# An attention and two gated layers on one core: the take of step 3 by halves, an earlier release of head B's tail, and the waits for values in another place

## The chip, the core and the metric

One core of one Trainium2 chip. Its engines work side by side: TensorE (matrix products into PSUM), VectorE, ScalarE, GpSimd, and SyncE, which issues the DMAs. They are kept in order by semaphores that the program sets and waits for. The metric is the device time in microseconds of one execution; lower is better. PSUM has 8 banks of 512 float32 for each of the 128 partitions.

## The reference

Three layers. The first takes almost half of the time and is the one that the change touches.

```python
q_pool = q.reshape(B, H, S // 2, 2, D).mean(axis=3)     # B 4, H 8, S 1152, D 64: 576 queries
scores = scale * (q_pool @ k.T)                         # 576 x 1152 a head
attn = exp(scores - max(scores)); attn /= sum(attn) + 1e-9
x = attn @ v
# layer 2: gelu(x @ w_in) split in u and v, v normalized and mixed over tokens, x + (u * v_s) @ w_out
# layer 3: token mixing and channel mixing with relu, both added to x
```

All is float32. Where a product must be exact, each operand is split in a high and a low part, and three products are summed.

## The kernel before, in words

The 32 heads are worked on in 16 pairs, called blocks here (index i, block 0 to 15); the pair's heads are A and B. A head has 576 queries: four tiles of 128 and a tail of 64. The two tails of a pair make one tile together, so a block has 9 tiles, one for each step s: steps 0 to 3 are the tiles of head A, step 4 (TAIL_STEP) is the joint tail, steps 5 to 8 are the tiles of head B. Blocks 1 to 14 run in a hardware loop whose body holds two of them on TensorE; block 15 is written out, and so is a rest of four steps, called block 16 here.

In each step TensorE does three things in this order (`step` in the TensorE program, L780):

- 18 transposes (L704, `transpose_p`) of the normalized probabilities of the tile that is 4 steps back (LAG), into banks 4 to 6. They wait until GpSimd has normalized that tile and until ScalarE and VectorE have copied the previous transposes out of the banks.
- The product with V (L775, `values`) for the pair before, spread over the steps by PV_STEPS: blocks of 128 keys, 9 for head A in steps 0 to 3 (3, 2, 2, 2) and 9 for head B in steps 4 to 8 (1, 2, 2, 2, 2). Each block of keys is two matmuls, each of which shows as two passes. They sum up in bank 7.
- The scores of this step's tile (`scores`, L759, and for the tail L742 to L744) into banks 0 to 3, 288 keys a bank. They wait for `s_taken`: VectorE has taken the scores of the step before out of these banks. For the tail there are 12 matmuls over the whole array, three for each bank in turn, elsewhere 24 on half of it, two at a time.

VectorE has in each step: the copy of half of the transposes (L1329, `evac_p`), the reciprocal of the sum of the tile two steps back (L1320, L1322), and the take (L1313, `take`): one operation of 128x1152 that scales the scores, writes them to `prob` and reduces them to the negated row maximum in `nmax`; the accumulated value is written by a small second instruction, which also reports `s_taken`. ScalarE copies the other half of the transposes and those of the last block of keys (L1081), does the exponential with `nmax` as bias (L1095) and copies the sums of the value product to `xT`. GpSimd normalizes (L592) and prepares q and k of the next block (L552 to L585); late in blocks 13 to 15 it also splits the first weights of layer 2. SyncE issues the loads, V among them (L459), and the copies of q and k to the other half of the partitions.

The transposed probabilities `pT` are held once for each head. Before they are overwritten, `pT_free` (L425) waits for `acc_ready`, which the last block of keys in `values` reports. For the tail of head B, in step 8, both VectorE (all blocks of keys but the last) and ScalarE (the last) wait in this way.

The first block of keys in a head's `values` stands behind four waits: the accumulator is copied out (`acc_moved`), the transposes of all tiles of the head are copied by VectorE and by ScalarE (`pT_by_dve`, `pT_by_act`), and V is there (`v_in`). In the loop the counts of such waits depend on the block and are worked out by instructions of TensorE's queue.

In block 0, steps 0 to 3 use the banks 0 to 3 and 4 to 7 in turn, and the transposes of its step 4 wait for all four takes.

Of the kernel before, what the change touches and what calls it, by code (L numbers as in the profile page):

```python
# [54 lines left out]
def build(nc, q, k, v, x_w_in, g_ln, w_sg, b_sg, w_out, w_tok1, w_tok2, w_ch1, w_ch2, out):  # L55
# [49 lines left out]
    def sem(name):  # L105
        return top.enter_context(nc.semaphore(name))

    with top:
# [31 lines left out]
        ctx0.close()  # L140
        pT = sb(ctx1, "pT", [P, 2, KB, SQ])
        nmax = sb(ctx1, "nmax", [P, NS])
        esum = sb(ctx1, "esum", [P, NS])
        lsum = sb(ctx1, "lsum", [P, NS])
        rsum = sb(ctx1, "rsum", [P, NS])
# [88 lines left out]

        s_ready = sem("s_ready")
        s_taken = sem("s_taken")
        exp_done = sem("exp_done")
        lsum_ready = sem("lsum_ready")
        rsum_ready = sem("rsum_ready")
# [2 lines left out]
        pT_by_act = sem("pT_by_act")  # L242
        pT_by_dve = sem("pT_by_dve")
        acc_ready = sem("acc_ready")
        acc_moved = sem("acc_moved")

        sgT_hi = sem("sgT_hi")
# [435 lines left out]
        def _(pe):  # L683
# [39 lines left out]
            def scores(i, par, s, first):  # L723

                zero = isinstance(i, int) and i == 0
                if s == (TAIL_STEP if zero else 0):
                    pe.wait_ge(q_split, at(i, 1, 1))
                    pe.wait_ge(k_split, at(i, 1, 1))
                if s == 0 and not zero:
                    pe.wait_ge(over_put[0], at(i, 64, 0))  # L730
                if s == TAIL_STEP + 1:
                    pe.wait_ge(over_put[1], at(i, 64, 64))
                if first and s < LAG:
                    if s >= 2:
                        pe.wait_ge(s_taken, s - 1)
                else:
                    pe.wait_ge(s_taken, at(i, NS, s))
                if s == TAIL_STEP:
                    tail = slice(4 * P, QC)
                    for c in range(SCORE_BANKS):  # L740
                        cols = slice(c * CK, (c + 1) * CK)
                        te.matmul(ps[:, c, 0:CK], qh2[:, par, tail], kh2[:, par, cols], start=True, stop=False)  # L742
                        te.matmul(ps[:, c, 0:CK], qh2[:, par, tail], kl2[:, par, cols], start=False, stop=False)  # L743
                        ins = te.matmul(ps[:, c, 0:CK], ql2[:, par, tail], kh2[:, par, cols], start=False, stop=True)  # L744
                        if c >= 2:
                            ins.then_inc(s_ready, 1)
                    return
                a, q0 = head_of(s), tile_of(s) * P
                b0 = first_bank(s) if first else 0
                for m in range(2):  # L750
                    if s == 0 and zero:
                        pe.wait_ge(two_split, 2 + m)
                    if s == 2 and zero:
                        pe.wait_ge(q_rest_split, 1)
                    for term in range(3):
                        for t in range(2):
                            wh, wl, xh, xl = row_tile(i, a, t, par, q0, 2 * m + t)
                            w, x = ((wh, xh), (wh, xl), (wl, xh))[term]
                            ins = te.matmul(ps[:, b0 + 2 * m + t, 0:CK], w, x, start=(term == 0), stop=(term == 2))  # L759
                            if m == 1 and term == 2:  # L760
                                ins.then_inc(s_ready, 1)

            def values(i, a, js):

                if js[0] == 0:
                    if not (isinstance(i, int) and i + a == 0):
                        pe.wait_ge(acc_moved, at(i, 4, 2 * a))
                    last = TAIL_STEP if a == 0 else NS - 1
                    pe.wait_ge(pT_by_dve, at(i, NS, last + 1))
                    pe.wait_ge(pT_by_act, at(i, 2 * NS, 2 * last + 2))  # L770
                    pe.wait_ge(v_in[a], at(i, 16, 16))
                n = HALF
                for j in js:
                    for c in range(2):
                        ins = te.matmul(ps[PH * c:PH * c + PH, ACC_BANK, 0:n], v_sb[:, a, j, :],  # L775
                                        pT[:, a, j, c * n:c * n + n], start=(j == 0), stop=(j == KB - 1))
                        if j == KB - 1:
                            ins.then_inc(acc_ready, 1)

            def step(i, par, s, first=False, tail=False):  # L780

                if s >= LAG and not tail:
                    if first and s == LAG:
                        pe.wait_ge(s_taken, LAG)
# [168 lines left out]
            pe.wait_ge(w_split, U_WO)  # L953
            v_tile(0, 0)
            v_tile(0, 1)
            for s in range(TAIL_STEP, NS):
                values(NP - 1, *PV_STEPS[s])
            for b in range(B):
# [316 lines left out]
        def _(dve):  # L1275
# [29 lines left out]
            def take(i, s):  # L1305
# [3 lines left out]
                if not (isinstance(i, int) and i + before[0] < 0):  # L1309
                    dve.wait_ge(p_ready, at(i + before[0], 2 * NS, 2 * before[1] + 2))  # L1310
                dve.wait_ge(s_ready, at(i, 2 * NS, 2 * s + 2))
                b0 = first_bank(s) if isinstance(i, int) and i == 0 else 0
                ve.tensor_scalar(prob[:, PROB_BUF[s], :].rearrange("p (c n) -> p c n", c=SCORE_BANKS),  # L1313
                                 ps[:, b0:b0 + SCORE_BANKS, 0:CK], -SCALE, BIG, ALU.mult, ALU.min,
                                 accum_out=nmax[:, s:s + 1]).then_inc(s_taken, 1)
# [8 lines left out]
            def evac_p(i, s):  # L1324

                dve.wait_ge(p_ready, at(i, 2 * NS, 2 * s + 2))
                if s in (0, TAIL_STEP, TAIL_STEP + 1):
                    pT_free(dve, i, head_of(s))
                ve.tensor_copy(pT_of(s, 1), trans(1)).then_inc(pT_by_dve, 1)  # L1329

            def step(i, s, first=False, tail=False):
# [274 lines left out]
```

## Time and profile before

| what | us |
|---|---|
| median of 3 runs | 1007.95 (1007.74 to 1008.92) |
| the profiled execution | 1007.09 |
| its span | 1005.0 |
| TensorE busy in the span | 985.4 (98%), 8898 matmuls |
| VectorE busy | 568.5 (57%) |
| ScalarE busy | 464.0 (46%) |
| GpSimd busy | 382.8 (38%) |

The profiled execution is one, and its span begins and ends a little inside its time. Matmuls overlap one another, so a busy TensorE isn't one without gaps: what counts is when a group of matmuls starts after the one before it. The attention lasts until about 429 us; from there on TensorE works on layers 2 and 3. The granted clock of TensorE is 9 tenths or more in every slice but the first (8 tenths).

### The profile page before, as it was taken

What the parts mean: (1) busy time and instruction counts of PE and PEld (TensorE: products, weight loads), DVE (VectorE), ACT (ScalarE), POOL (GpSimd) and SP (SyncE); (2) the same over time, 40 slices, a digit from 0 to 9 for tenths busy, and PEclk for the clock granted to TensorE, in tenths of its full rate; (3) what the DMA queues carried; (4) which work ended last, traced back from release to release, by engine and by line L of the source; (5) the groups of instructions that cost most, each with busy time, mean ns of one, the idle gap of its engine ahead of it and who ended that gap; (6) DMA issues with size and microseconds to landing.
All of it is one profiled execution on the core that took longest, in us unless ns stands there. A gap on an engine that the chain in (4) does not pass through costs nothing.

```text
span 1005.0 us, 22892 instructions
## 1 busy us (share of the span) xinstructions
PE 985.4 (98%) x8898; PEld 813.9 (81%) x8898; DVE 568.5 (57%) x1125; ACT 464.0 (46%) x880; POOL 382.8 (38%) x297
## 2 busy tenths in 40 slices
PE   6999999999999999999999999999999999999998
PEld 6877777777777777679999999988888888888898
DVE  6777777777777777779484948554213113121121
ACT  4787777777777877754242514222111111111111
POOL 4877777777777777730000104385000000000000
PEclk8999999999999999999999999999999999999999
DMA  5644444444444434310000000142001001000010
GB/s 184 182 119 118 117 117 117 116 112 114 116 117 117 117 91 109 111 55 1 1 2 1 2 1 24 46 135 73 1 0 42 1 1 42 0 15 27 0 42 22
DMA packets 34475, 65.55 MB, mean 65 GB/s; under 512 B 6272, under 2 KB 15360, under 8 KB 34432
## 3 DMA queue, kind: packets, MB, share of 16 engines
q1 hardware_dynamic: 33984, 64.37, 22.5%
q8 instruction: 33, 0.54, 0.2%
q10 hardware_dynamic: 448, 0.56, 0.2%
q14 instruction: 10, 0.08, 0.0%
HBM read 42.93 MB, written 4.72 MB: 47 GB/s over the span
## 4 chain that ended last, share of the span: by engine, by line
PE 92%; issue 2%; DVE 2%; POOL 1%; ACT 1%; DMA 1%; SPq 0%; DVEq 0%; ACTq 0%; POOLq 0%
PE ps L816 18%; PE ps L817 18%; PE ps L818 18%; PE ps L775 14%; PE ps L759 11%; PE ps L704 7%; PE ps L742 1%; DVE prob L1313 1%; PE ps L743 1%; PE ps L744 1%; PE ps L868 1%; DMA k_raw<-in_k 1%; ACT prob L1095 1%; POOL prob L592 0%; PE ps L822 0%
## 5 line engine op out<-in xcount | busy, mean ns | idle before, releaser
L1313 DVE TENSOR_SCALAR_CACHE_REDUCE prob<-ps 128x1152 f32<-128x1152 f32 x144 | 195.4, 1358 | 82.0 <-PE ps L759 62.8
L592 POOL TENSOR_SCALAR prob<-prob,rsum 128x1152 f32<-128x1152 f32 x144 | 178.4, 1239 | 106.0 <-DVE rsum L1322 106.0
L1095 ACT ACTIVATE prob<-prob,nmax 128x1152 f32<-128x1152 f32 x144 | 181.2, 1258 | 5.2
L775 PE MATMUL ps<-pT,v_sb 128*64 128x288 f32 x1152 | 170.6, 418 | 1.3
L1554 DVE SCALAR_TENSOR_TENSOR f_l<-ps,f_h 128x512 fp32r<-128x512 f32 (+1 forms) x60 | 38.3, 638 | 222.4 <-ACT f_h L1262 222.4
L1262 ACT ACTIVATE f_h<-ps 128x512 fp32r<-128x512 f32 (+1 forms) x60 | 33.3, 555 | 254.7 <-PE ps L818 254.7
L1081 ACT ACTIVATE pT<-ps 128x512 f32<-128x512 f32 (+1 forms) x288 | 111.9, 435 | 78.0 <-PE ps L704 69.4
L759 PE MATMUL ps<-k_over,q_over 64*128 64x288 f32 x744 | 131.5, 309 | 0.0
L759 PEld LDWEIGHTS ps<-k_over,q_over 64*128 64x128 f32 x744 | 102.1, 184 | 26.4 <-DVE prob L1313 25.8
L704 PE MATMUL ps<-ident,prob 64*128 64x64 f32 x2592 | 106.8, 224 | 6.7 <-DVE prob L1313 3.9
L704 PEld LDWEIGHTS ps<-ident,prob 64*128 64x128 f32 x2592 | 100.7, 139 | 13.8 <-issue 12.8
L1329 DVE COPY pT<-ps 128x512 f32<-128x512 f32 x144 | 98.9, 687 | 10.3 <-PE ps L775 5.7
L775 PEld LDWEIGHTS ps<-pT,v_sb 128*64 128x64 f32 x1152 | 70.8, 136 | 40.9 <-issue 3.2
L817 PE MATMUL ps<-u_l,c_h 128*128 128x512 f32 (+1 forms) x240 | 88.3, 368 | 0.0
L816 PE MATMUL ps<-u_h,c_h 128*128 128x512 f32 (+1 forms) x240 | 88.3, 368 | 0.0
L818 PE MATMUL ps<-u_h,c_l 128*128 128x512 f32 (+1 forms) x240 | 88.3, 368 | 0.0
L816 PE MATMUL ps<-f_h,c_h 128*128 128x512 f32 (+1 forms) x240 | 88.3, 368 | 0.0
L817 PE MATMUL ps<-f_l,c_h 128*128 128x512 f32 (+1 forms) x240 | 88.3, 368 | 0.0
L818 PE MATMUL ps<-f_h,c_l 128*128 128x512 f32 (+1 forms) x240 | 88.3, 368 | 0.0
L759 PE MATMUL ps<-kh,qh 64*128 64x288 f32 x248 | 85.3, 344 | 0.6 <-DMA k_over<-kl 0.6
L652 POOL TENSOR_TENSOR rstd<-var_e,minus_half 128x1 f32<-128x1 f32 x18 | 13.3, 741 | 167.2 <-DVE var_e L1405 167.2
L759 PE MATMUL ps<-kl,qh 64*128 64x288 f32 x248 | 72.3, 291 | 0.0
(156 smaller groups left out, 2136.9 us busy)
## 6 DMA issues: line engine op xcount, KB each, us to landing
q_raw<-in_q SPq DMA_DIRECT2D x16, 640.0 KB, 5.2
k_raw<-in_k SPq DMA_DIRECT2D x16, 576.0 KB, 4.0
v_sb<-in_v SPq DMA_DIRECT2D x32, 288.0 KB, 2.9
k_over<-kh SPq DMA_DIRECT2D x31, 144.0 KB, 2.5
k_over<-kl SPq DMA_DIRECT2D x31, 144.0 KB, 2.6
out_x<-xT SPq DMA_DIRECT2D x4, 1024.0 KB, 4.2
q_over<-qh SPq DMA_DIRECT2D x31, 128.0 KB, 2.2
q_over<-ql SPq DMA_DIRECT2D x31, 128.0 KB, 2.3
```

The costliest lines, as they stand in the source:

```text
L592: g.tensor_scalar(sl, sl, rsum[:, s:s + 1], 0.0, ALU.mult, ALU.add).then_inc(norm_done, 1)
L704: ins = te.transpose(dst, prob[half, PROB_BUF[s], j * P:(j + 1) * P], ident[half, half])
L759: ins = te.matmul(ps[:, b0 + 2 * m + t, 0:CK], w, x, start=(term == 0), stop=(term == 2))
L775: ins = te.matmul(ps[PH * c:PH * c + PH, ACC_BANK, 0:n], v_sb[:, a, j, :], pT[:, a, j, c * n:c * n + n], start=(j == 0), stop=(j == KB - 1))
L816: te.matmul(acc, wh, xh, start=start, stop=False)
L817: te.matmul(acc, wh, xl, start=False, stop=False)
L818: return te.matmul(acc, wl, xh, start=False, stop=stop)
L1081: return sc.activation(o, i_, ACT.Copy)
L1095: sc.activation(sl, sl, ACT.Exp, scale=-1.0, bias=nmax[:, s:s + 1], accum_out=esum[:, s:s + 1]).then_inc(exp_done, 1)
L1313: ve.tensor_scalar(prob[:, PROB_BUF[s], :].rearrange("p (c n) -> p c n", c=SCORE_BANKS), ps[:, b0:b0 + SCORE_BANKS, 0:CK], -SCALE, BIG, AL ...
L1329: ve.tensor_copy(pT_of(s, 1), trans(1)).then_inc(pT_by_dve, 1)
L1554: ve.scalar_tensor_tensor(out=f_l[:, f % F_N, 0:n], in0=ps[:, f % F_N, 0:n], scalar=0.0, in1=f_h[:, f % F_N, 0:n].bitcast(F32), op0=ALU.ma ...
```

## The change

- The take of step 3 is done in two operations of 128x576, two banks each. Each reports `half_taken` and leaves its own negated maximum in `nmax_half`. VectorE then waits for both and joins them with one scalar operation of 128x1 (the minimum of the two) into `nmax`, which reports `s_taken`.
- The scores of the tail (step 4) no longer wait for `s_taken`; they wait for the first half ahead of bank 0 and for the second ahead of bank 2.
- In step 8 VectorE's copy of the tail of head B waits for `tail_read`, which `values` reports when the eighth block of keys (number 7) of head B is done, and no longer for the ninth. ScalarE's copy waits as before.
- The wait for V of a head stands at the start of step 0 or 4, ahead of the transposes, and the two waits for `pT_by_dve` and `pT_by_act` in `values` are left out; behind the loop, ahead of the last values, the three stand written out.

```diff
--- before.py
+++ after.py
@@ -140,6 +140,7 @@
         ctx0.close()
         pT = sb(ctx1, "pT", [P, 2, KB, SQ])
         nmax = sb(ctx1, "nmax", [P, NS])
+        nmax_half = sb(ctx1, "nmax_half", [P, 2])
         esum = sb(ctx1, "esum", [P, NS])
         lsum = sb(ctx1, "lsum", [P, NS])
         rsum = sb(ctx1, "rsum", [P, NS])
@@ -234,6 +235,7 @@
 
         s_ready = sem("s_ready")
         s_taken = sem("s_taken")
+        half_taken = sem("half_taken")
         exp_done = sem("exp_done")
         lsum_ready = sem("lsum_ready")
         rsum_ready = sem("rsum_ready")
@@ -242,6 +244,7 @@
         pT_by_act = sem("pT_by_act")
         pT_by_dve = sem("pT_by_dve")
         acc_ready = sem("acc_ready")
+        tail_read = sem("tail_read")
         acc_moved = sem("acc_moved")
 
         sgT_hi = sem("sgT_hi")
@@ -733,11 +736,13 @@
                 if first and s < LAG:
                     if s >= 2:
                         pe.wait_ge(s_taken, s - 1)
-                else:
+                elif s != TAIL_STEP:
                     pe.wait_ge(s_taken, at(i, NS, s))
                 if s == TAIL_STEP:
                     tail = slice(4 * P, QC)
                     for c in range(SCORE_BANKS):
+                        if c % 2 == 0:
+                            pe.wait_ge(half_taken, at(i, 2, c // 2 + 1))
                         cols = slice(c * CK, (c + 1) * CK)
                         te.matmul(ps[:, c, 0:CK], qh2[:, par, tail], kh2[:, par, cols], start=True, stop=False)
                         te.matmul(ps[:, c, 0:CK], qh2[:, par, tail], kl2[:, par, cols], start=False, stop=False)
@@ -765,10 +770,6 @@
                 if js[0] == 0:
                     if not (isinstance(i, int) and i + a == 0):
                         pe.wait_ge(acc_moved, at(i, 4, 2 * a))
-                    last = TAIL_STEP if a == 0 else NS - 1
-                    pe.wait_ge(pT_by_dve, at(i, NS, last + 1))
-                    pe.wait_ge(pT_by_act, at(i, 2 * NS, 2 * last + 2))
-                    pe.wait_ge(v_in[a], at(i, 16, 16))
                 n = HALF
                 for j in js:
                     for c in range(2):
@@ -776,9 +777,14 @@
                                         pT[:, a, j, c * n:c * n + n], start=(j == 0), stop=(j == KB - 1))
                         if j == KB - 1:
                             ins.then_inc(acc_ready, 1)
+                        elif j == KB - 2 and a == 1 and c == 1:
+                            ins.then_inc(tail_read, 1)
 
             def step(i, par, s, first=False, tail=False):
 
+
+                if s in (0, TAIL_STEP) and not first:
+                    pe.wait_ge(v_in[s // TAIL_STEP], at(i, 16, 0))
                 if s >= LAG and not tail:
                     if first and s == LAG:
                         pe.wait_ge(s_taken, LAG)
@@ -953,6 +959,9 @@
             pe.wait_ge(w_split, U_WO)
             v_tile(0, 0)
             v_tile(0, 1)
+            pe.wait_ge(pT_by_dve, NP * NS)
+            pe.wait_ge(pT_by_act, NP * 2 * NS)
+            pe.wait_ge(v_in[1], NP * 16)
             for s in range(TAIL_STEP, NS):
                 values(NP - 1, *PV_STEPS[s])
             for b in range(B):
@@ -1310,6 +1319,16 @@
                     dve.wait_ge(p_ready, at(i + before[0], 2 * NS, 2 * before[1] + 2))
                 dve.wait_ge(s_ready, at(i, 2 * NS, 2 * s + 2))
                 b0 = first_bank(s) if isinstance(i, int) and i == 0 else 0
+                if s == TAIL_STEP - 1:
+
+                    for m in range(2):
+                        cols = slice(m * 2 * CK, (m + 1) * 2 * CK)
+                        ve.tensor_scalar(prob[:, PROB_BUF[s], cols].rearrange("p (c n) -> p c n", c=2),
+                                         ps[:, b0 + 2 * m:b0 + 2 * m + 2, 0:CK], -SCALE, BIG, ALU.mult, ALU.min,
+                                         accum_out=nmax_half[:, m:m + 1]).then_inc(half_taken, 1)
+                    dve.wait_ge(half_taken, at(i, 2, 2))
+                    ve.tensor_scalar(nmax[:, s:s + 1], nmax_half[:, 0:1], nmax_half[:, 1:2], None, ALU.min).then_inc(s_taken, 1)
+                    return
                 ve.tensor_scalar(prob[:, PROB_BUF[s], :].rearrange("p (c n) -> p c n", c=SCORE_BANKS),
                                  ps[:, b0:b0 + SCORE_BANKS, 0:CK], -SCALE, BIG, ALU.mult, ALU.min,
                                  accum_out=nmax[:, s:s + 1]).then_inc(s_taken, 1)
@@ -1324,8 +1343,11 @@
             def evac_p(i, s):
 
                 dve.wait_ge(p_ready, at(i, 2 * NS, 2 * s + 2))
-                if s in (0, TAIL_STEP, TAIL_STEP + 1):
+                if s in (0, TAIL_STEP + 1):
                     pT_free(dve, i, head_of(s))
+                if s == TAIL_STEP and not (isinstance(i, int) and i == 0):
+
+                    dve.wait_ge(tail_read, at(i, 1, 0))
                 ve.tensor_copy(pT_of(s, 1), trans(1)).then_inc(pT_by_dve, 1)
 
             def step(i, s, first=False, tail=False):
```

## Rows read from the trace of the kernel before

**Rows 1.** the page, part 4 (the chain that ended last, shares of the span)

```profile
PE 92%; issue 2%; DVE 2%; POOL 1%; ACT 1%; DMA 1%; SPq 0%; DVEq 0%; ACTq 0%; POOLq 0%
```

**Rows 2.** timeline of TensorE, a regular step (start us, us, engine, line, op, tiles)

```profile
207.43 0.40 PE L759 MATMUL ps<-k_over,q_over 64*128 64x288 f32 x1
...
208.33 0.71 PE L704 MATMUL ps<-ident,prob 64*128 64x64 f32 x18
208.98 1.19 PE L775 MATMUL ps<-pT,v_sb 128*64 128x288 f32 x8
210.10 0.40 PE L759 MATMUL ps<-k_over,q_over 64*128 64x288 f32 x1
```

**Rows 3.** timeline of TensorE, steps 3 to 5 of one block

```profile
198.59 0.40 PE L759 MATMUL ps<-kh,qh 64*128 64x288 f32 x1
...
199.49 0.72 PE L704 MATMUL ps<-ident,prob 64*128 64x64 f32 x18
200.34 0.71 PE L775 MATMUL ps<-pT,v_sb 128*64 128x288 f32 x4
201.15 0.40 PE L742 MATMUL ps<-kh,qh 128*128 128x288 f32 x1
...
202.93 0.77 PE L704 MATMUL ps<-ident,prob 64*128 64x64 f32 x18
```

**Rows 4.** timeline of TensorE, step 8 of that block to step 0 of the next

```profile
212.76 0.40 PE L759 MATMUL ps<-k_over,q_over 64*128 64x288 f32 x1
...
213.77 0.77 PE L704 MATMUL ps<-ident,prob 64*128 64x64 f32 x18
214.48 1.68 PE L775 MATMUL ps<-pT,v_sb 128*64 128x288 f32 x12
216.09 0.39 PE L759 MATMUL ps<-kh,qh 64*128 64x288 f32 x1
```

**Rows 5.** timeline of VectorE, steps 3 and 4, and the tail's copy in step 8

```profile
199.73 1.36 DVE L1313 TENSOR_SCALAR_CACHE_REDUCE prob<-ps 128x1152 f32<-128x1152 f32 x1 [0.45 <-PE ps L759]
201.01 0.08 DVE L1313 DVE_READ_ACCUMULATOR prob<-ps 128x1 f32 x1
201.01 0.69 DVE L1329 COPY pT<-ps 128x512 f32<-128x512 f32 x1
201.61 0.15 DVE L1320 TENSOR_SCALAR lsum<-esum 128x1 f32<-128x1 f32 x1
...
203.04 1.36 DVE L1313 TENSOR_SCALAR_CACHE_REDUCE prob<-ps 128x1152 f32<-128x1152 f32 x1 [1.08 <-PE ps L744]
...
212.97 0.69 DVE L1329 COPY pT<-ps 128x512 f32<-128x512 f32 x1 [0.38 <-PE ps L775]
```

**Rows 6.** timeline of TensorE, step 4 of block 15

```profile
407.72 0.40 PE L742 MATMUL ps<-kh,qh 128*128 128x288 f32 x1 [0.29 <-DVE prob L1313]
```

**Rows 7.** list of waits (us in total, times, longest us)

```profile
DVE pT L1329 <- PE ps L775: 5.7, 15, 0.4
```

**Rows 8.** timelines of ScalarE and of GpSimd, in the same block

```profile
201.59 1.26 ACT L1095 ACTIVATE prob<-prob,nmax 128x1152 f32<-128x1152 f32 x1
...
212.91 0.28 ACT L1081 ACTIVATE pT<-ps 128x128 f32<-128x128 f32 x1 [0.53 <-PE ps L775]
...
203.28 1.25 POOL L592 TENSOR_SCALAR prob<-prob,rsum 128x1152 f32<-128x1152 f32 x1
```

**Rows 9.** timeline of SyncE's queue, step 3

```profile
198.87 0.33 SPq L459 DMA_DIRECT2D v_sb<-in_v  x1
```

**Rows 10.** timeline of TensorE, step 0 of block 1

```profile
37.39 0.39 PE L759 MATMUL ps<-kh,qh 64*128 64x288 f32 x1 [0.63 <-DMA k_over<-kl]
```

**Rows 11.** the chain in order of time, block 0 (start us, us, what)

```profile
14.97 1.28 DVE prob L1313 x2
```

**Rows 12.** timelines of GpSimd and of TensorE, block 13 to step 2 of block 14

```profile
367.27 1.23 POOL L592 TENSOR_SCALAR prob<-prob,rsum 128x1152 f32<-128x1152 f32 x1 [0.89 <-DVE rsum L1322]
...
373.82 0.78 PE L704 MATMUL ps<-ident,prob 64*128 64x64 f32 x18 [0.83 <-POOL prob L592]
```

## The prediction

> **What bounds the kernel now.** I read the page first: TensorE holds 92% of the chain that ended last [rows 1], so only TensorE's own gaps are worth anything, and a gap that comes back once per block of the attention counts 15 times (blocks 1 to 15; block 0 is filled differently). The timeline of TensorE shows the regular step: first score matmul 207.43, transposes 208.33, values 208.98, next scores 210.10 [rows 2]. That is 0.90, 0.65 and 1.12, a step of 2.67. Two places in a block leave this grid.
>
> Step 3 to step 4: scores 198.59, transposes 199.49, values 200.34, tail scores 201.15 [rows 3]. Transposes to values is 0.85 instead of 0.65, values to scores 0.81. Step 4 has only 4 value passes: 12 passes take 216.09 - 214.48 = 1.61 [rows 4] where 8 take 1.12 [rows 2], so 4 passes are 0.49 and 4 passes before scores should take 1.12 - 0.49 = 0.63. The whole stretch is 2.56; on the grid it would be 0.90 + 0.65 + 0.63 = 2.18.
>
> Step 8 to step 0: scores 212.76, transposes 213.77, values 214.48 [rows 4]: 1.01 and 0.71 instead of 0.90 and 0.65. The 1.61 behind them is on the grid.
>
> Who holds these gaps? For step 4 VectorE's rows say it: the take of step 3 runs from 199.73, its accumulator read ends at 201.01 + 0.08 = 201.09 [rows 5], and the tail scores start 0.06 later. The four waits in front of the values (0.20 late) are at present covered by it: in block 15 the row of the tail scores names the take as releaser too [rows 6]. Either edit alone would give little or only a part there: without the take the values' waits still cost 0.20. For step 0 it is VectorE's copy of head B's tail at 212.97 [rows 5]: it ends at 213.66, the transposes that overwrite its bank begin at 213.77. The list of waits has that copy held back by a value matmul 15 times, 5.7 us in all [rows 7].
>
> **Take by halves.** 1152 elements occupy VectorE 201.01 - 199.73 = 1.28, 512 occupy it 201.61 - 201.01 = 0.60 [rows 5]: 0.68 for 640, so 1.06 ns each and 0.06 fixed. A half of 576 is then about 0.67 to 0.68. First half: 199.73 + 0.68, its read 0.08, 0.06 to TensorE: 200.55. TensorE wants its banks at 198.59 + 2.18 = 200.77: 0.22 to spare. Second half: 199.73 + 1.36 + 0.08 + 0.06 = 201.23. Bank 2 is wanted after six tail matmuls; twelve and the switch behind them take 202.93 - 201.15 = 1.78 [rows 3], so not before 200.77 + 0.8 = 201.57: 0.34 to spare. If the second half must wait for the first one's read (0.08) both still hold. No row has two accumulating operations back to back; I bound the extra cost of a half from nothing to that of a whole further small operation with its read, 0.06 to 0.3, and take 0.08, which the rows of the copy beside the read show.
>
> The joining operation is a 128x1 one like lsum: 0.15 [rows 5], with its start some 0.18. So the maximum of step 3 is 0.08 + 0.08 + 0.18, at most some 0.35 later, as is all that VectorE does behind it: the copy for step 0's transposes ends at 201.70 + 0.35 = 202.05, and the transposes of step 5 come at 202.93 - 0.38 = 202.55. Behind it the two small operations end by 202.35, the take of step 4 can start no earlier than 203.04 - 0.38 = 202.66 [rows 5]. ScalarE's exponential of step 3 starts at 201.59 before [rows 8], later than the new maximum (201.44). GpSimd's normalization 203.28 to 204.53 [rows 8] sits behind a split that starts from step 3, not from step 4, so it doesn't move; its transposes are two steps on, at 205.66 - 0.38 = 205.28 on the grid. Nothing comes late. Taken with the next edit the stretch goes from 2.56 to 2.18. I take 0.37, a little under the 0.38, for the blocks not shown: 15 x 0.37 = **5.6 off**. The ends for this term: 0.2 (if the halves are 0.17 later than I reckon) to 0.38 a block.
>
> **Waits for values.** The two waits for the transposed blocks are covered, since the transposes of the same step wait for a later copy; the wait for V goes ahead of the transposes, where TensorE's queue is still full of scores. Queued behind it are the transposes. V for head A is issued at 198.87 [rows 9] and lands in 2.9 by the page's median; wanted at 213.6. It never bites. Per wait removed from the short stretch between transposes and values I count the 0.20 above over three, and none left: in block 15, whose counts are constants, nothing of the kind shows before the take's row. Its gain is in the 0.37 already. Alone it is nothing, for the take would still end at 201.09.
>
> **Head B's tail.** VectorE's copy only waits for block 7 of head B. The eight passes of step 8 end at 212.83, and block 8 is the last four of them, 0.49 earlier: 212.35. VectorE is free at 212.59, its read ends there. So the copy starts at about 212.55, 0.42 earlier, and ends at 213.24. Next late would be ScalarE's copy 212.91 to 213.19 [rows 8], which still waits for block 8; the transposes are due at 212.76 + 0.90 = 213.66. So 1.01 becomes 0.90. The 0.06 behind it (transposes that start into an idle array) should go as well: 0.17. At every other boundary the loop branches back and the new wait stands right behind the branch: I take 0.12 there, so 0.15 on average (bounds 0 to 0.22). Not all boundaries pay:
> - Into block 1 it is lost: TensorE then waits 0.63 for a DMA of the k copies [rows 10].
> - Into blocks 2 to 13: 12 x 0.15 = **1.8 off**.
> - Into blocks 14 and 15 TensorE stands later on GpSimd, which splits a weight in between (0.83 before the transposes at 373.82). That chain starts with the normalization at 367.27, for which GpSimd had waited 0.89 on VectorE's reciprocal behind this very copy [rows 12]. A copy 0.42 earlier starts it 0.42 earlier: 2 x 0.42 = **0.8 off**.
> - Into block 16 ScalarE's chain from the end of block 8 decides, which isn't moved: nothing.
>
> **Block 0** has the take of step 3 on its chain (14.97, followed by the preparation of q [rows 11]), and its transposes wait for the whole take in any case: 0.3 longer (0.25 to 0.4), passed on to the scores that wait in [rows 10]: **0.3 on**.
>
> The Trainium skill, "Perfetto Trace Analysis", section "Optimizing Scalar/DVE Operations", gives VectorE some 125 ns of access per instruction that reads PSUM, against the 60 to 80 of the rows. By it each half costs 0.05 more, block 0 loses 0.4 and the sum changes by 0.1; the same section allows breaking up an instruction where the engine has slack but makes another one wait, and here VectorE stands idle for 1.08 before the take at 203.04 [rows 5].
>
> **Sum.** 5.6 + 1.8 + 0.8 - 0.3 = 7.9 off. The profiled execution took 1007.09 (span 1005.0 and 2.1 around it): 999.2. The median of the runs shown is 1007.95, 0.86 above it; with the same distance the time is **1000.1**. Behind the attention everything hangs on its end and shifts as a whole.
>
> **Rivals.**
> 1. The halves come late. For: no row of such a pair, only 0.22 to spare. Against: every part of it has a row. At 0.17 beyond the spare time step 4 gives 0.2: 15 x 0.17 = 2.6 less, **1002.7**. Chance 0.10.
> 2. The tail's edit gives nothing. For: ScalarE's copy of the last block ends at 213.19, and both engines must have reported; the branch. Against: 0.47 lies between it and the transposes on the grid (213.66). Then 1.8 and 0.8 go: **1002.7**. Chance 0.10. If only the boundaries with the branch fail: 1000.9, within my own range.
> 3. It doesn't do what it says: the tail scores start where they did, because their second half's wait or another operand holds them; only the tail's edit counts, less block 0: 1007.95 - 2.3 = **1005.6**. For: nothing in the rows. Chance 0.05.
> 4. Slower: VectorE becomes what TensorE waits for at step 5. There the transposes need VectorE's copy behind the take, at present 202.93 - 201.70 = 1.23 apart, 0.85 on the new grid. If two halves, two reads and the join take x longer than one take, this decides from x = 0.85, and cancels the gains of a block (0.53) at x = 1.4. With x = 1.7 a block is 0.3 longer: 15 x 0.3 = 4.5, block 0 pays the 1.7 in full, the 0.8 of blocks 14 and 15 stays: 1007.95 + 5.4, **1013**. For: an accumulating operation may have a cost that only shows when another follows. Against: five times my 0.34. Chance 0.04.
>
> The forecast holds the remaining 0.71, with its own range 998.9 to 1001.3 (boundary term 0 to 2.6, block 0). The range for 8 in 10 reaches to the rivals at 1002.7: **998.5 to 1003.3**. No change can be told within about 0.2% (2.0 us): faster by more than that is the forecast, rivals 1 and 2 and nearly all of 3, less a little for what I have not seen: 0.91; within 0.2%: 0.05; slower: 0.04.
>
> **What will show it.** Tail scores 2.18 behind the scores of step 3 (2.56 now); transposes to values in step 4 0.65; VectorE's rows with two 128x576 takes of about 0.76 and a 128x1 operation; the copy of the tail right behind the take, and no row left that waits for a value matmul there; transposes of step 0 0.90 to 0.95 behind the scores; TensorE's waits of 0.83 in block 14 about 0.4 shorter. A block takes 25.0 instead of 25.5. I am wrong if the tail scores still start at the end of the (second) take, if transposes of step 5 wait for VectorE, or if the block stays above 25.2.

## The result and the profile after

The changed kernel takes 999.52 us (median of 5 runs, 998.60 to 1003.18), the kernel before 1008.92 (5 runs, 1007.74 to 1010.57): a ratio of 0.9918, interval 0.9902 to 0.9935 (the two medians by themselves give 0.9907, inside it). In a second comparison it was 0.9922 [0.9905, 0.9940]. The forecast was 1000.1, which is 0.9922 of the 1007.95 it started from.

The chain of the page (part 4), beside [rows 1]:

```profile
PE 94%; DVE 1%; POOL 1%; ACT 1%; issue 1%; DMA 1%; SPq 0%; ACTq 0%; DVEq 0%; POOLq 0%
```

Timeline of TensorE, steps 3 to 5 of the same block as in [rows 3], and step 8 to step 0 as in [rows 4] (L764 scores, L707 transposes, L776 values, L747 tail scores):

```profile
198.26 0.40 PE L764 MATMUL ps<-kh,qh 64*128 64x288 f32 x1
...
199.16 0.71 PE L707 MATMUL ps<-ident,prob 64*128 64x64 f32 x18
199.81 0.71 PE L776 MATMUL ps<-pT,v_sb 128*64 128x288 f32 x4
200.44 0.40 PE L747 MATMUL ps<-kh,qh 128*128 128x288 f32 x1
...
202.23 0.78 PE L707 MATMUL ps<-ident,prob 64*128 64x64 f32 x18
...
212.06 0.40 PE L764 MATMUL ps<-kh,qh 64*128 64x288 f32 x1
...
212.96 0.72 PE L707 MATMUL ps<-ident,prob 64*128 64x64 f32 x18
213.62 1.68 PE L776 MATMUL ps<-pT,v_sb 128*64 128x288 f32 x12
```

Both places are on the grid now: 0.90, 0.65, 0.63 make 2.18 from the scores of step 3 to the tail scores (2.56 before), and step 8 to step 0 is 0.90 and 0.66 (1.01 and 0.71 before). VectorE in the same block, beside [rows 5] (L1326 the halves, L1330 the join, L1351 the copy):

```profile
199.39 0.76 DVE L1326 TENSOR_SCALAR_CACHE_REDUCE prob<-ps 128x576 f32<-128x576 f32 x1 [0.44 <-PE ps L764]
200.07 0.08 DVE L1326 DVE_READ_ACCUMULATOR prob<-ps 128x1 f32 x1
200.07 0.75 DVE L1326 TENSOR_SCALAR_CACHE_REDUCE prob<-ps 128x576 f32<-128x576 f32 x1
200.75 0.08 DVE L1326 DVE_READ_ACCUMULATOR prob<-ps 128x1 f32 x1
200.87 0.21 DVE L1330 TENSOR_SCALAR nmax<-nmax_half 128x1 f32<-128x1 f32 x1
201.00 0.68 DVE L1351 COPY pT<-ps 128x512 f32<-128x512 f32 x1
...
202.34 1.36 DVE L1332 TENSOR_SCALAR_CACHE_REDUCE prob<-ps 128x1152 f32<-128x1152 f32 x1 [0.40 <-PE ps L749]
...
211.81 0.08 DVE L1332 DVE_READ_ACCUMULATOR prob<-ps 128x1 f32 x1
211.81 0.69 DVE L1351 COPY pT<-ps 128x512 f32<-128x512 f32 x1
```

A half occupies VectorE 0.68, the second starts with the read of the first. The copy starts 1.61 behind the start of the take, 1.28 before. The tail's copy (211.81) starts with the accumulator read. The wait of [rows 7] is gone from the list of waits, and so is nearly all of the issue time of TensorE's weight loads (PEld) ahead of the values (3.2 us in 15 times before):

```profile
PEld ps L776 <- issue: 0.4, 1, 0.4
```

To compare kernels I use the start of the tail scores in each block. The first two rows are of before (block 1, block 13), the next two of after:

```profile
47.95 0.40 PE L742 MATMUL ps<-kh,qh 128*128 128x288 f32 x1
354.33 0.40 PE L742 MATMUL ps<-kh,qh 128*128 128x288 f32 x1
```

```profile
50.69 0.40 PE L747 MATMUL ps<-kh,qh 128*128 128x288 f32 x1
350.22 0.40 PE L747 MATMUL ps<-kh,qh 128*128 128x288 f32 x1
```

| stretch, us | before | after | difference |
|---|---|---|---|
| start to tail scores of block 1 | 47.95 | 50.69 | +2.74 |
| block 1 to block 13 (12 blocks) | 306.38 | 299.53 | -6.85 |
| block 13 to 14 | 26.53 | 25.72 | -0.82 |
| block 14 to 15 | 26.85 | 26.29 | -0.57 |
| block 15 to the end of the span | 597.25 | 597.17 | -0.08 |
| span | 1005.0 | 999.4 | -5.6 |

The profiled execution of after took 1001.20, 1.7 above its median, and the first row says where. The windows view (stretch, us, busy time of PE, PEld, DVE, ACT, POOL, granted clock as a share of 2.4 GHz, DMA share and GB/s) of before, then of after:

```profile
18.00:24.00 6.00, 5.28 (x48) 5.00 (x48) 2.86 (x6) 1.66 (x4) 3.47 (x3) 0.59 0.77 214
24.00:32.00 8.00, 8.00 (x150) 7.86 (x146) 6.83 (x15) 6.94 (x13) 5.80 (x4) 1.00 0.78 282
```

```profile
18.00:24.00 6.00, 4.72 (x26) 4.44 (x27) 3.40 (x6) 1.78 (x4) 4.02 (x4) 0.53 0.73 213
24.00:32.00 8.00, 8.00 (x91) 7.96 (x90) 3.49 (x11) 3.90 (x9) 3.52 (x3) 0.50 0.82 288
```

In block 0 TensorE runs at 1.2 GHz for a time, after a stretch in which it was mostly idle; in this execution of after it went on until some 32 us, in that of before until some 23.

### The profile page after: what moved, and what is told of

Same layout as the page of the kernel before. It is cut to its first block, busy times and chain, and to the rows that moved or that the text cites. A ratio compares the mean times of both kernels' runs of the same rounds, so it can differ in the third digit from the quotient of the medians.

```text
span 999.4 us, 22942 instructions
## 1 busy us (share of the span) xinstructions
PE 983.6 (98%) x8898; PEld 816.6 (82%) x8898; DVE 571.4 (57%) x1173; ACT 463.9 (46%) x880; POOL 383.1 (38%) x297
## 4 chain that ended last, share of the span: by engine, by line
PE 94%; DVE 1%; POOL 1%; ACT 1%; issue 1%; DMA 1%; SPq 0%; ACTq 0%; DVEq 0%; POOLq 0%
PE ps L822 18%; PE ps L824 18%; PE ps L823 18%; PE ps L776 15%; PE ps L764 12%; PE ps L707 8%; PE ps L747 1%; PE ps L749 1%; PE ps L748 1%; PE ps L874 1%; DVE prob L1332 1%; POOL prob L595 0%; DMA k_two<-in_k 0%; PE ps L828 0%; PE ps L829 0%
## 5 line engine op out<-in xcount | busy, mean ns | idle before, releaser
L1332 DVE TENSOR_SCALAR_CACHE_REDUCE prob<-ps 128x1152 f32<-128x1152 f32 x128 | 173.7, 1358 | 68.8 <-PE ps L764 60.2
L776 PE MATMUL ps<-pT,v_sb 128*64 128x288 f32 x1152 | 170.6, 418 | 0.0
L764 PE MATMUL ps<-k_over,q_over 64*128 64x288 f32 x744 | 132.7, 311 | 0.0
L764 PEld LDWEIGHTS ps<-k_over,q_over 64*128 64x128 f32 x744 | 103.3, 187 | 26.3 <-DVE prob L1332 25.8
L707 PE MATMUL ps<-ident,prob 64*128 64x64 f32 x2592 | 106.7, 224 | 5.8 <-DVE nmax L1330 3.3
L707 PEld LDWEIGHTS ps<-ident,prob 64*128 64x128 f32 x2592 | 102.0, 139 | 10.3 <-issue 10.3
L1351 DVE COPY pT<-ps 128x512 f32<-128x512 f32 x144 | 98.7, 686 | 6.9 <-PE ps L707 6.9
L776 PEld LDWEIGHTS ps<-pT,v_sb 128*64 128x64 f32 x1152 | 70.2, 136 | 39.0 <-issue 0.4
L764 PE MATMUL ps<-kh,qh 64*128 64x288 f32 x248 | 85.9, 347 | 0.2 <-DMA k_over<-kl 0.2
L764 PE MATMUL ps<-kh,ql 64*128 64x288 f32 x248 | 72.9, 294 | 0.0
```

Of the source, the lines that this page charges most:

```text
L707: ins = te.transpose(dst, prob[half, PROB_BUF[s], j * P:(j + 1) * P], ident[half, half])
```

## The experiments

In each, the stretch of 12 blocks is read from the profile (tail scores of block 1 to those of block 13); it repeats within 0.1 us for one kernel (299.53 and 299.57 for the changed kernel, taken twice).

| kernel | 12 blocks | median us | ratio to before |
|---|---|---|---|
| before | 306.38 | 1008.20, 1008.77 | 1 |
| halves alone | 303.65 | 1006.35 | 0.998 [0.9969, 0.999] |
| tail alone | 304.55 | 1005.93 | 0.998 [0.997, 0.9989] |
| waits alone | 306.21 | 1007.23 | 0.9996 [0.9986, 1.0006] |
| halves and waits | 302.13 | 1003.39 | 0.995 [0.9931, 0.997] |
| all three | 299.57 | 1000.34 | 0.9922 [0.9905, 0.994] |

The kernel before was run beside them each time: 1008.20 is its median beside the first four, 1008.77 beside the last. Edits of the first four: parts of the diff shown above, on the kernel before.

**Halves alone.**

```diff
+                        if c % 2 == 0:
+                            pe.wait_ge(half_taken, at(i, 2, c // 2 + 1))
```

> Only the take of step 3 by halves; values keep their four waits, the tail of head B its late release. Theory (take and waits hide each other): values still start 0.80 to 0.85 behind the transposes of step 4, the tail scores follow 0.63 later, so the stretch from the scores of step 3 to the tail scores is 2.34 to 2.38 instead of 2.56 (before) and 2.18 (all three edits): 0.2 off a block, 12 blocks from the tail scores of block 1 to those of block 13 shorter by 2.2 to 2.4. Rival (the take alone held the stretch): 2.18 and 4.5 off over the 12 blocks. Block 0 0.3 to 0.6 longer by both. Time about 3 below before, against 5 by the rival.

Timeline of TensorE (L706 transposes, L779 values, L746 tail scores):

```profile
198.06 0.40 PE L763 MATMUL ps<-kh,qh 64*128 64x288 f32 x1
...
198.95 0.72 PE L706 MATMUL ps<-ident,prob 64*128 64x64 f32 x18
199.75 0.71 PE L779 MATMUL ps<-pT,v_sb 128*64 128x288 f32 x4
200.39 0.40 PE L746 MATMUL ps<-kh,qh 128*128 128x288 f32 x1
```

The tail scores no longer wait for the take (0.64 behind the values), but the values are 0.80 behind the transposes: 2.33 in all. The 12 blocks are 2.73 shorter, 0.23 a block, a little more than the 2.2 to 2.4 expected. The theory holds, the rival (4.5) falls. The median is 1.9 lower, not the 3 expected.

Block 15 of the same run is a control. It stands outside the loop, so the counts of its waits are constants and nothing has to be worked out for them. There the values come 0.65 behind the transposes and the stretch is 2.18, with the four waits in place. So the waits as such cost nothing there; what costs time in the loop goes with counts that have to be worked out.

**Tail alone.**

```diff
-                if s in (0, TAIL_STEP, TAIL_STEP + 1):
+                if s in (0, TAIL_STEP + 1):
                     pT_free(dve, i, head_of(s))
+                if s == TAIL_STEP and not (isinstance(i, int) and i == 0):
+                    dve.wait_ge(tail_read, at(i, 1, 0))
```

> Only the earlier release of head B's tail to VectorE's copy. Theory: scores of step 8 to transposes of step 0 0.90 instead of 1.01 and 1.05; transposes to values 0.65 instead of 0.71 if that 0.06 came from a start into an idle array. 12 blocks 2.0 to 2.4 shorter, block 14 0.3 to 0.4; time about 2.5 below before. Rival (the 0.06 behind it and the loop branch come from the waits of the values): 0.71 stays, and where the loop branches back 0.95 to 1.0; 12 blocks 1.2 shorter.

```profile
264.85 0.40 PE L760 MATMUL ps<-k_over,q_over 64*128 64x288 f32 x1
...
265.76 0.72 PE L705 MATMUL ps<-ident,prob 64*128 64x64 f32 x18
266.45 1.68 PE L776 MATMUL ps<-pT,v_sb 128*64 128x288 f32 x12
```

The transposes come on time at every boundary (0.90 to 0.91, where the loop branches back too), but within the loop the values stay 0.69 to 0.75 behind them. The 12 blocks are 1.83 shorter. Neither side was wholly right: the loop's branch costs nothing (theory), but the values don't come earlier (rival), although the transposes now start on time. Into block 15, whose waits have constant counts, they do: 0.65.

**Waits alone.**

```diff
-                    pe.wait_ge(pT_by_dve, at(i, NS, last + 1))
-                    pe.wait_ge(pT_by_act, at(i, 2 * NS, 2 * last + 2))
-                    pe.wait_ge(v_in[a], at(i, 16, 16))
+                if s in (0, TAIL_STEP) and not first:
+                    pe.wait_ge(v_in[s // TAIL_STEP], at(i, 16, 0))
```

> Only the waits: V's ahead of the transposes, the two for the transposed blocks left out. Theory: in step 4 transposes to values falls from 0.80 to 0.85 to 0.65, but values to tail scores grows from 0.85 to 1.00, the tail scores stay tied to the end of the take: 2.55 as before, no gain there, the time as before within 0.1%. Rival (the waits also cost in step 0): transposes to values there 0.65 instead of 0.71, 12 blocks 0.7 shorter.

```profile
198.46 0.40 PE L759 MATMUL ps<-kh,qh 64*128 64x288 f32 x1
...
199.35 0.72 PE L704 MATMUL ps<-ident,prob 64*128 64x64 f32 x18
200.00 0.71 PE L771 MATMUL ps<-pT,v_sb 128*64 128x288 f32 x4
201.00 0.40 PE L742 MATMUL ps<-kh,qh 128*128 128x288 f32 x1 [0.29 <-DVE prob L1314]
```

The values move up by 0.15 to 0.20 and the tail scores don't follow: 2.54, tied to the take. No change of the time can be told (0.17 in the 12 blocks). In step 0 the transposes are still late, and the values 0.70 to 0.71 behind them (0.71 to 0.76 with the waits). So two causes hide each other there too. Late transposes without the waits (this run) give 0.70 to 0.71, the waits behind transposes that are on time (the run before this one) 0.69 to 0.75, and with neither it is 0.64 to 0.66 at nearly all boundaries of after. The forecast's cause, transposes that start late, and the rival's, the waits, are both there.

**Halves and waits.**

> Take by halves and the waits, without the tail's release. Theory: step 3 to step 4 2.18, all of the changed kernel's gain there; step 8 to step 0 as before (1.01 to 1.05, then 0.71). 12 blocks 4.4 shorter, against 6.85 measured for all three edits. Rival (the edits help each other at the block boundary as well): more than 4.8.

The 12 blocks are 4.26 shorter, 0.355 a block: step 4 is on the grid (2.18), the boundary as before. The rival (more than 4.8) falls. The tail's edit on top of these two is worth 2.56, against 1.83 by itself.

**The changed kernel again, and block 0.** The second kernel keeps one take in block 0:

```diff
-                        if c % 2 == 0:
-                            pe.wait_ge(half_taken, at(i, 2, c // 2 + 1))
+                        if c % 2 == 0 and not zero:
+                            pe.wait_ge(half_taken, at(i, 2, c // 2 - 1))
-                if s == TAIL_STEP - 1:
+                if s == TAIL_STEP - 1 and not (isinstance(i, int) and i == 0):
...
-                    dve.wait_ge(half_taken, at(i, 2, 2))
+                    dve.wait_ge(half_taken, at(i, 2, 0))
```

> The changed kernel once more, beside three kernels made from it. Theory: its blocks are fixed (299.5 from the tail scores of block 1 to those of block 13, within 0.1), and what varies is block 0, where TensorE's granted clock stays at 1.2 GHz for a shorter or longer stretch: the tail scores of block 1 anywhere from 48 to 51. Rival: the longer block 0 (50.7 against 47.9 before) belongs to the change, and every execution shows it.

> The changed kernel, but in block 0 the take of step 3 stays one operation (its transposes wait for all of it anyway). Theory: from the start of that take to the start of the low part of q 1.97 as before instead of 2.28, so 0.3 less in block 0 and nothing elsewhere; too little for the medians. Rival: the stretch at 1.2 GHz comes from the halves, then the tail scores of block 1 come at 48 instead of 50.7 and the time falls by about 2.5.

The same program reached the tail scores of block 1 at 48.61 this time (50.69 in the first profile), with 299.57 for the 12 blocks. So most of the longer block 0 is no property of the change. The kernel with the tail's edit alone, which has no halves, had 50.21, and the slow clock until about 31. With the whole take in block 0: 47.92. The stretch from the start of that take to the low part of q is 2.05 instead of 2.36 (14.83 to 16.88, against 15.01 to 17.37), the 0.3 that was forecast. The medians, 1000.05 and 1000.34, can't tell it, and no run shows that the halves lengthen the slow stretch.

Behind that stretch more than 0.3 is lost, which the profiles show side by side. In six of them the full clock was back by 24 us. Three have no halves in block 0 (before, waits alone, whole take in block 0) and reach the tail scores of block 1 at 47.95, 47.89 and 47.92. Three have them (halves alone, the changed kernel again, and the kernel with three small operations below) and reach them at 48.54, 48.61 and 48.56. That is 0.6 to 0.7. The take's own rows show 0.3 of it; where the rest is lost isn't shown.

**GpSimd's splitting of weights moved.** It needs no part of the change.

```diff
-            body(NP - 3, 1, w0=0, w=(7, 8))
-            body(NP - 2, 0, w0=1, w=(7, 8))
-            body(NP - 1, 1, last=True, w0=2, w=(0, 2, 4, 6))
+            body(NP - 3, 1, w0=0, w=(5, 6))
+            body(NP - 2, 0, w0=1, w=(5, 6))
+            body(NP - 1, 1, last=True, w0=2, w=(2, 3, 5, 6))
```

> The changed kernel, with GpSimd's splitting of the first weights moved: in blocks 13 and 14 to steps 5 and 6 (was 7 and 8), in block 15 to steps 2, 3, 5 and 6 (was 0, 2, 4, 6). Theory: what is left of the waits on GpSimd goes, 0.69 in block 14 (scores of step 1 to transposes of step 2 0.90 instead of 1.59) and 1.26 in block 15 (step 2 to 3, 0.90 instead of 2.16), because GpSimd is idle for 1.6 and 1.4 in steps 5 and 6: 1.9 to 2.0 below the changed kernel, blocks 14 and 15 25.0 each. Rival: the split pushes the normalizations behind it, and the transposes of step 0 come late instead: under 1.0 gained.

From tail scores to tail scores, block 13 to 14 and 14 to 15 take 24.95 and 24.97: 2.4 less than in the profile beside it (25.69 and 26.63), 2.1 less than in the first (25.72 and 26.29), where 1.9 to 2.0 was expected. The two late places that the expectation names are on the grid. The median is 998.81 against 1000.34, but the intervals of the two ratios overlap (0.9883 to 0.9917, 0.9905 to 0.9940), so the profile shows this gain and the medians don't separate it. GpSimd around the boundary of blocks 13 and 14:

```profile
358.38 2.40 POOL L603 TENSOR_TENSOR wi_l<-stage,wi_h 128x1024 fp32r<-128x1024 f32 x1
360.75 1.23 POOL L595 TENSOR_SCALAR prob<-prob,rsum 128x1152 f32<-128x1152 f32 x1
362.52 1.23 POOL L595 TENSOR_SCALAR prob<-prob,rsum 128x1152 f32<-128x1152 f32 x1 [0.54 <-DVE rsum L1341]
```

GpSimd waits for VectorE again (0.54) before the second of these normalizations: the split in front of the first no longer makes it late.

**Both of the former.**

> Both of the former edits on the changed kernel. Theory: they add up, 2.2 to 2.4 below the changed kernel, about 997.3, 10.5 below the kernel before. Rival (one of them gives nothing): 999.

996.75 (996.09 to 999.38), ratio 0.9885 [0.9867, 0.9903]: the lowest median of all, 12.0 below the kernel before and 3.6 below the changed one, though the interval overlaps those of the neighbours. Its 12 blocks are 299.50, the two stretches behind them 24.97 and 24.95, so the gains at the end of the attention are all there. Whether the two edits add up in the time isn't shown: the fall of the median is larger than the 2.2 to 2.4 expected, while the execution that was profiled was the slowest of the five (slow clock until 31, and 598.1 from the tail scores of block 15 to the end, where most profiles have 597.2).

**How much more VectorE could bear behind the halves.** Additions ahead of the join, used by nothing:

```diff
+                    for n in range(3):     # 7 in the second
+                        ve.tensor_tensor(pad[:, n * P:(n + 1) * P], ident[:, :], ident[:, :], ALU.add)
                     dve.wait_ge(half_taken, at(i, 2, 2))
```

> The changed kernel with three additions of 128x128 on VectorE ahead of the join of the halves (their result is used by nothing): some 0.6 longer in step 3. Read from the blocks 1 to 13. Theory (the spare time behind the take is 0.54: copy for step 0's transposes ends at 201.68, transposes of step 5 at 202.22): just used up, 0 to 0.15 longer a block, 299.5 to 301.3. The tail scores stay 2.18 behind the scores of step 3, since they wait for the halves and not for the join. Rival (VectorE's delay reaches the next steps through the takes): all of 0.6 a block, 306.7.

> The same with seven additions: some 1.4 longer. Theory: 1.4 less 0.54 spare, 0.85 to 0.9 longer a block, all of it ahead of the transposes of step 5 (scores of step 4 to transposes 2.65 instead of 1.79); 12 blocks 309.7 to 310.3, slower than the kernel before (306.4): the point from which the change turns slower lies between three and seven additions. Rival (the take of step 4, late too, adds its own delay to the scores of step 5): more than 311.

Each was run once. The 12 blocks are 326.35 and 347.35 (1032.23 and 1058.75 us), far beyond both sides. The tail scores stayed 2.18 behind. The expected length of the additions was wrong. VectorE of the first, and GpSimd in the same stretch:

```profile
212.49 2.78 DVE L1331 TENSOR_TENSOR pad<-ident 128x128 f32<-128x128 f32 x3
215.20 0.20 DVE L1333 TENSOR_SCALAR nmax<-nmax_half 128x1 f32<-128x1 f32 x1
...
212.06 2.67 POOL L589 TENSOR_TENSOR kl<-k_raw,kh 128x1152 fp32r<-128x1152 f32 x1
```

The three take 2.78, not 0.6: the first ends 0.14 behind GpSimd's operation (212.06 + 2.67 = 214.73), the others take 0.20 each. They read two SBUF operands each, and the first waits for GpSimd's operation to end. Rows of the kernel before show the same where nothing was added, in block 0, for VectorE's sum of q and for its low part of q (two SBUF operands each), with GpSimd beside them:

```profile
13.05 1.93 DVE L1298 TENSOR_TENSOR q_sum<-q_raw 128x640 f32<-128x640 f32 x1
16.94 1.73 DVE L1303 TENSOR_TENSOR ql<-q_sum,qh 128x640 fp32r<-128x640 f32 x1
```

```profile
11.65 2.64 POOL L585 TENSOR_TENSOR kl<-k_raw,kh 128x1152 fp32r<-128x1152 f32 x1 [1.85 <-ACT kh L1081]
16.69 1.31 POOL L592 TENSOR_SCALAR prob<-prob,rsum 128x1152 f32<-128x1152 f32 x1 [0.62 <-DVE rsum L1322]
```

They end at 14.98 and 18.67, GpSimd's at 14.29 and 18.00: 0.69 and 0.67 behind, whenever they began. The second shows that one operand on GpSimd's side is enough. Where GpSimd had just ended (whole take in block 0), the sum of q took 0.81.

The join moved by 2.59. A block grew by 2.11 in eleven of the twelve (27.05 to 27.10 instead of 24.96) and by 3.6 in the other, block 8: there the granted clock fell to 1.2 GHz from 243.0 to 246.5, in a pause of TensorE of 2.06 ahead of the transposes of step 5. With seven additions the pause is 2.86, and the clock falls in seven of the twelve blocks. One of these, TensorE and VectorE in block 6, and the windows view:

```profile
196.19 1.23 PE L708 MATMUL ps<-ident,prob 64*128 64x64 f32 x18 [2.84 <-issue]
197.35 2.19 PE L777 MATMUL ps<-pT,v_sb 128*64 128x288 f32 x8
199.46 0.61 PE L765 MATMUL ps<-k_over,q_over 64*128 64x288 f32 x1
```

```profile
196.30 1.36 DVE L1335 TENSOR_SCALAR_CACHE_REDUCE prob<-ps 128x1152 f32<-128x1152 f32 x1
197.58 0.08 DVE L1335 DVE_READ_ACCUMULATOR prob<-ps 128x1 f32 x1
```

```profile
196.00:202.00 6.00, 5.81 (x56) 4.36 (x56) 3.12 (x9) 2.87 (x6) 2.45 (x2) 0.50 0.57 163
```

The values take 2.19 instead of 1.19, which puts the scores of step 5 up to 1.0 late. The take of step 4 had been over since 197.66, so it isn't what they wait for. In the five blocks at the full clock these scores are on time, and a block grew by 2.91, with a join 3.38 later. So the rival's mechanism (the take adds its own delay) doesn't show; the average of 3.98 a block is 2.91 and the clock.

To have additions that GpSimd doesn't hold, I tried operations of one operand:

```diff
+                    for n in range(3):     # 12 in the second
+                        ve.tensor_scalar(pad[:, n:n + 1], ident[:, 0:1], 1.0, None, ALU.add)
```

> The changed kernel with three operations of 128x1 with one operand ahead of the join (used by nothing), some 0.13 each, 0.4 together. Unlike the additions of two operands they should not be held by GpSimd's split of k. Theory (0.54 to spare between VectorE's copy and the transposes of step 5): nothing lost, 12 blocks 299.5 to 299.7. Rival (VectorE's operations are held in that place whatever they are): 2.2 a block as with three additions, 326.

> The same with twelve: 1.5 to 1.6 together. Theory: what goes beyond 0.54 is lost once a block, ahead of the transposes of step 5: 1.0 a block, 12 blocks 311 to 312.5, slower than the kernel before (306.4); scores of step 4 to transposes of step 5 2.75 to 2.85. Rival (the take of step 4 adds its own delay to the scores behind it): more than 314.

Each was run once. Three: 299.56, nothing lost, as the theory has it; the rival falls. GpSimd's split of k ran beside them (198.21 to 200.88, the three from 198.64) and didn't hold them. They differ from the additions in size too (128x1 against 128x128), and a large operation of one operand in this place wasn't tried. Twelve: 301.39. They start 0.06 apart, not 0.13, so the join moved by only 0.61, and a block grew by 0.153. The expected 311 is missed for that reason, and this run says nothing of a change that turns slower than before. VectorE and TensorE of the twelve:

```profile
200.30 0.81 DVE L1331 TENSOR_SCALAR pad<-ident 128x1 f32<-128x1 f32 x12
201.03 0.20 DVE L1333 TENSOR_SCALAR nmax<-nmax_half 128x1 f32<-128x1 f32 x1
201.16 0.68 DVE L1354 COPY pT<-ps 128x512 f32<-128x512 f32 x1
```

```profile
201.94 0.77 PE L708 MATMUL ps<-ident,prob 64*128 64x64 f32 x18
```

The transposes follow the copy's end (201.84) by 0.10. So the time to spare is 0.61 - 0.15 = 0.46. Three and seven additions give the same in the blocks at the full clock, 2.59 - 2.11 = 0.48 and 3.38 - 2.91 = 0.47. What goes beyond it is lost one for one, until the pause that it makes brings the clock down as well.

## Why the prediction was right

- **Step 4**, 0.37 a block: right, by place and by size. 0.355 measured by itself in the 12 blocks. As forecast it rests on two causes that hide each other: 0.23 and 0.01 alone, 0.355 together.
- **The halves' price**: 0.08 + 0.08 + 0.18 = up to 0.35 estimated, 0.33 measured (1.61 - 1.28). The read of the first half does not hold the second. The estimate worked out from the figure in the Trainium skill ("Perfetto Trace Analysis", "Optimizing Scalar/DVE Operations") would have been 0.05 more for each half; here the rows of the kernel before were the better source.
- **Waits for values**: no gain alone, right. But the working had their effect in step 4 only. At the boundary the forecast put the 0.06 down to late transposes alone (a start into an idle array), and the runs show the waits to be a second cause, which remains once the transposes are on time.
- **The boundary**, 0.15 a block: mis-sized. 0.21 to 0.22 measured on top of the other two edits (2.56 / 12). The 0.12 for boundaries with the loop's branch was an unneeded deduction: they gain more than the others (scores to transposes from 1.05 to 0.91, against 1.01 to 0.90).
- **Blocks 14 and 15**, 0.42 each beside step 4: 0.45 in block 14 (0.82 less 0.37), right and by the mechanism named: GpSimd's wait of [rows 12] fell from 0.89 to 0.42. TensorE's wait fell from 0.83 to 0.54, by 0.3 and not by the 0.4 forecast, since TensorE itself comes to this place earlier, by what the boundary gained. In block 15 0.20: there the step failed. The chain doesn't start from the normalization but from SyncE, which issues the load of the next weights behind the copies of q and k; GpSimd waits for that DMA. The rows of after (GpSimd, block 14 to 15):

```profile
391.98 1.23 POOL L595 TENSOR_SCALAR prob<-prob,rsum 128x1152 f32<-128x1152 f32 x1
395.82 1.05 POOL L555 TENSOR_SCALAR wi_h<-stage 128x1024 fp32r<-128x1024 f32 x1 [2.60 <-DMA stage<-in_moe_w_in]
```

  The wait grew from 2.35 to 2.60, as GpSimd arrives earlier and the DMA doesn't: SyncE issues it 15.87 behind the tail scores of block 14 in both kernels. Block 14 to 15 was 26.29, 26.63 and 26.39 in three profiles of the same body: a landing decides.
- **Block 0**, 0.3: right by the rows of the chain (17.50 - 15.22 = 2.28 against 16.94 - 14.97 = 1.97), too small for the block as a whole, where the profiles show 0.6 to 0.7. What the forecast didn't have either is that block 0 varies with TensorE's clock: by 2.1 us between two profiles of the changed kernel (50.69 and 48.61).
- **The sum**: 7.9 forecast. Without block 0 the profile shows 6.85 + 0.82 + 0.57 + 0.08 = 8.3 and the 0.37 of block 1, less 0.3 to 0.7: 8.0 to 8.4. The ratio says 8.3. The boundary term was too small by 0.7, and step 4, block 15 and block 0 came out some 0.2 or more worse than forecast, so errors partly cancel. That the time itself came within 0.6 is in part luck, since the medians of one kernel move by almost 1 between comparisons (999.52 and 1000.34; 1008.20 to 1008.92).
- **Rivals**: 1 and 3 fall by the row of the tail scores, 2 by the transposes of step 0. Rival 4, the slower one, is a real mechanism, though not what happened: the tests with additions put its start at 0.46 to 0.48 more of VectorE's time (0.50 by the forecast's 0.85 less its 0.35), and with 2.6 more the kernel is far slower than before.

## What to carry to other kernels

Where an engine's gap has two causes that end at nearly the same time, take both away together: alone, one edit looked worthless and the other worth two thirds of what both give. Split an operation of the feeding engine so that its consumer can start on the first part, if the rows show idle time behind it for the added reads and join; look at what GpSimd does in that very place before you put any operation of two SBUF operands on VectorE there. To compare such kernels use a stretch of regular work in the profile: it repeats within 0.1 us, where single executions of one kernel scatter by 3 to 6 and their medians by almost 1. When such a stretch grows more than it should, look at each block and at its granted clock before you name a wait.

## What the runs showed of the hardware

- An addition of two SBUF operands on VectorE (128x128, 0.20 by itself) took 2.38 while GpSimd ran an operation of 2.67, and ended 0.14 behind it. VectorE's operations of two SBUF operands of 128x640 ended 0.67 to 0.69 behind GpSimd's, and one operand on GpSimd's side was enough. Additions of one operand of 128x1, accumulating takes from PSUM and copies from PSUM ran beside GpSimd's operation of two operands at their usual time.
- Two accumulating takes back to back start 0.68 apart at 576 elements (1.28 at 1152); the accumulator's read costs no time of its own between them.
- Three waits whose counts are worked out for the block made TensorE 0.15 to 0.20 late between transposes and values, where little is queued ahead. With constant counts (block 15) the same waits cost nothing there, and the one that was moved ahead of the transposes, where scores are queued, shows no cost either.
- In block 0 the granted clock fell to 1.2 GHz in every profile, at 15.4 to 18.4 us, with TensorE busy for 1.1 to 2.5 of the 6 us from 12 to 18; it was back at between 22 and 32 us, by the execution. Where it was back by 25, the tail scores of block 1 came at 47.9 to 48.6 (49.0 and 49.3 in the kernels with seven and twelve additions); where it took until 28 to 32, at 49.8 to 50.7.
- In the loop a pause of TensorE of 2.06 in each block brought the clock down in one block of twelve, a pause of 2.86 in seven of twelve; the groups of matmuls behind it then took up to twice their time (values 2.19 instead of 1.19).
